# Attention tiles turned in 32x32 blocks on VectorE, one of six on TensorE, and the product with v in K=32 pieces

## The reference

```python
    q_bucket = np.sum(q_bits * powers, axis=-1)
    k_bucket = np.sum(k_bits * powers, axis=-1)
    mask = q_bucket[:, :, :, None] == k_bucket[:, :, None, :]
    scores = scale * np.matmul(q, k.transpose(0, 1, 3, 2))
    scores = np.where(mask, scores, -1000000000.0)
    scores = scores - np.max(scores, axis=-1, keepdims=True)
    attn = np.exp(scores)
    attn = attn / (np.sum(attn, axis=-1, keepdims=True) + 1e-09)
    return np.matmul(attn, v).astype(np.float32)
```

## Time and profile before

| | us |
|---|---|
| median of 3 runs (758.93 to 759.16) | 759.15 |
| the profiled execution | 759.28 |
| its span | 757.5 |
| TensorE busy | 747.0 (99%) |
| VectorE busy | 438.1 (58%) |
| ScalarE busy | 348.2 (46%) |
| GpSimd busy | 368.9 (49%) |

### The profile page before, as it was taken

One profiled execution on the slowest core, in us unless ns is written; L12 is line 12 of the kernel. 1 busy time (PEld: TensorE's weight loads), 2 busy tenths in 40 slices (PEclk: granted clock), 3 DMA queues, 4 the chain that ended last, 5 costly groups with the idle time before them and its releaser, 6 DMA issues.

```text
span 757.5 us, 12511 instructions
## 1 busy us (share of the span) xinstructions
PE 747.0 (99%) x4179; PEld 623.4 (82%) x4179; DVE 438.1 (58%) x858; ACT 348.2 (46%) x658; POOL 368.9 (49%) x253
## 2 busy tenths in 40 slices
PE   9999999999999999999999999999999999999996
PEld 7677777777776888888888888998899889889985
DVE  8777777777765745565555656597157027414710
ACT  7766677777764233432433310375057017404700
POOL 5966567878820799998978830253200120010001
PEclk9999999999999999999999999999999999999999
DMA  4434323212111799887886702510200010000000
GB/s 110 135 95 116 98 77 96 69 50 68 27 47 27 267 312 319 283 263 240 275 286 197 273 23 84 195 43 0 71 15 1 28 57 1 1 28 15 1 15 28
DMA packets 54301, 82.08 MB, mean 108 GB/s; under 512 B 21632, under 2 KB 33568, under 8 KB 54240
## 3 DMA queue, kind: packets, MB, share of 16 engines
q1 hardware_dynamic: 41152, 38.44, 16.8%
q10 hardware_dynamic: 9584, 31.53, 12.7%
q0 software_dynamic: 3504, 11.30, 4.6%
HBM read 64.67 MB, written 15.48 MB: 106 GB/s over the span
## 4 chain that ended last, share of the span: by engine, by line
PE 62%; issue 29%; POOL 3%; DVE 2%; ACT 2%; DMA 1%; SPq 0%; POOLq 0%; DVEq 0%
PE pair_s L1528 14%; PE pair_t L1543 14%; PE pair_u L1334 9%; PE bank_b L1349 8%; PE pair_s L1321 5%; PE pair_t L1321 4%; PE pair_u L1503 2%; PE bank_b L1374 2%; POOL out L682 1%; PE pair_s L1581 1%; DVE g_lo L1263 1%; PE pair_s L1454 1%; PE bank_a L1290 1%; POOL y_raw L676 1%; POOL w_part L550 1%
## 5 line engine op out<-in xcount | busy, mean ns | idle before, releaser
L550 POOL TENSOR_TENSOR w_part<-w_raw,w_part 128x1024 fp32r<-128x1024 f32 x80 | 190.5, 2404 | 45.9 <-ACT w_part L792 45.4
L792 ACT ACTIVATE w_part<-w_raw 128x1024 fp32r<-128x1024 f32 x72 | 76.3, 1060 | 117.8 <-DMA w_raw<-in_moe_w 102.9
L1630 PE MATMUL pair_t<-w_part,g_hi 128*128 128x512 f32 x384 | 119.0, 391 | 0.3 <-POOL w_part L550 0.3
L682 POOL DMA_INDIRECT out<-o_sb,token x12 | 11.8, 984 | 208.5 <-DVE o_sb L1233 208.5
L1528 PE MATMUL pair_s<-w_part,xs_t 128*128 x456 | 108.8, 394 | 0.2 <-issue 0.2
L1543 PE MATMUL pair_t<-w_part,hid_t 128*128 x456 | 107.1, 390 | 0.0
L1543 PEld LDWEIGHTS pair_t<-w_part,hid_t 128*128 128x128 f32 x456 | 85.4, 188 | 17.6
L1528 PEld LDWEIGHTS pair_s<-w_part,xs_t 128*128 128x128 f32 x456 | 84.3, 188 | 17.9 <-issue 0.9
L895 ACT ACTIVATE elu<-elu 128x384 f32<-128x384 f32 x64 | 33.6, 524 | 121.2 <-DVE elu L1253 121.1
L734 ACT ACTIVATE exps<-exps,nmax 128x768 f32<-128x768 f32 x96 | 88.5, 925 | 0.5 <-DVE exps L952 0.4
L1630 PEld LDWEIGHTS pair_t<-w_part,g_hi 128*128 128x128 f32 x384 | 71.6, 188 | 15.1 <-issue 0.7
(11 more groups left out here) (221 smaller groups left out, 1088.2 us busy)
## 6 DMA issues: line engine op xcount, KB each, us to landing
w_raw<-in_moe_w ACTq DMA_DIRECT2D x48, 512.0 KB, 3.9
w_raw<-in_moe_w SPq DMA_DIRECT2D x16, 512.0 KB, 8.1
ys_sorted<-ys SPq DMA_DIRECT2D x19, 256.5 KB, 6.4
x_sorted<-xs_raw SPq DMA_DIRECT2D x16, 256.0 KB
xs_q<-x_sorted SPq DMA_DIRECT2D x64, 64.0 KB, 4.7
w_raw<-in_moe_w_in ACTq DMA_DIRECT2D x8, 512.0 KB, 4.0
raw<-in_q SPq DMA_DIRECT2D x16, 192.0 KB, 3.2
raw<-in_k SPq DMA_DIRECT2D x16, 192.0 KB, 3.4
```

Of the source, the lines that this page charges most:

```text
L550: pool.tensor_tensor(chunk_of(w_part, n, 1, c), w_raw[n % 2][c][:, :], chunk_of(w_part, n, 0, c).bitcast(F32), ALU.subtract).then_inc(s_wl ...
L792: act.activation(chunk_of(w_part, n, 0, c), w_raw[n % 2][c][:, :], ACT.Copy).then_inc(s_whi, 1)
L1630: mm = pe.matmul(pair_t[:, t % 2, :], gp[:, f, j * P:(j + 1) * P], w_out_p[:, wp, f, :], start=f == 0 and m == 0, stop=f == FT - 1 and m == 2)
```

## The change

VectorE turns the first five tiles of each head itself, with one transpose instruction per tile, `turn(m)`, from `exps` to a new array `turned`. It transposes each 32x32 block in place, so that a partition holds key k of its block of 32 and every group of 32 partitions holds another quarter of the queries. The product with v therefore sums over 32 keys at a time: `times_v(u, first, end)` has for each pair of key blocks 4 row groups (one for each quarter, writing to a PSUM bank of its own) times 2 column groups, 96 products of K = 32 with 160 columns per head, in two pieces of 48 behind the first and the second score tile of the head two later. v is loaded four times per head in that layout (`v_quads`) and once as before.

The sixth tile is still turned by TensorE (`turn_alone`, into whichever score pair is free), copied whole by ScalarE (`copy_alone`), and multiplied by six products of 128 columns. In head 15 VectorE turns all six tiles, and the product comes in two parts (four tiles, two tiles). `last` has six products of 80 columns where it had three of 160. ScalarE takes over the rounding `high` for heads 3 and up, and no longer copies halves of turned tiles. Score pairs no longer alternate strictly, as `turn_alone` takes one in its turn. TensorE's scores are given tile by tile. The first product with v starts at m = 12, two heads behind the scores.

```diff
--- before.py
+++ after.py
+KEY_BLOCKS = S // 32
+PAIRS = KEY_BLOCKS // 2
+AV_AT = 512 - J * 32
+BLOCKED = J - 1
+ALONE_AT = AV_AT + 32 - P
...
-            v_nat = sb("v_nat", [P, 4, J, D])
             exps = sb("exps", [P, 4, S])
-            exps_t = sb("exps_t", [P, J, 4 * HALF])
+            turned = sb("turned", [P, 2 * BLOCKED + 1, S])
...
+            v_quads = sb("v_quads", [P, 3, KEY_BLOCKS * D])
+            v_nat = sb("v_nat", [P, 3, J, D])
...
+        quad = ctx.enter_context(nc.psum_tensor("quad", [P, 4, 512], F32))
         pair_s = ctx.enter_context(nc.psum_tensor("pair_s", [P, 2, 512], F32))
         pair_t = ctx.enter_context(nc.psum_tensor("pair_t", [P, 2, 512], F32))
-        pair_u = ctx.enter_context(nc.psum_tensor("pair_u", [P, 2, 512], F32))
+        bank_a, bank_b, pair_u = quad[:, 0, :], quad[:, 1, :], quad[:, 2:4, :]
...
+        scored = lambda m: score_pair[use_of(m) % 2]
+        alone = lambda h: score_pair[(use_of(J * (h + 1) + JH - 1) + 1) % 2]
+        first_turned = lambda u: 512 - blocked(u) * 32
+        out_pair = lambda u: pair_t if u == HEADS - 2 else quad[:, 1:3, :]
...
             def load_v(g):
-                if g >= 4:
+                if g >= 3:
                     sp.wait_ge(s_av, g - 2)
-                sp.dma_start(v_nat[:, g % 4], rows(v, g)).then_inc(s_vld[g % 4], 16)
+                for i in range(4):
+                    sp.dma_start(v_quads[i * 32:(i + 1) * 32, g % 3, :].rearrange("k (p n) -> k p n", p=4),
+                                 quad_rows(v, g)).then_inc(s_vld[g % 3], 16)
+                if g < HEADS - 1:
+                    sp.dma_start(v_nat[:, g % 3], rows(v, g)).then_inc(s_vld[g % 3], 16)
...
+            def high(g, c):
+                at = (slice(0, D), slice(D, P))[c]
+                if c == 0:
+                    act.wait_ge(s_raw[g % 2][0], 16 * (g // 2 + 1))
+                else:
+                    act.wait_ge(s_ks, g)
+                act.wait_ge(s_sc, J * (g - 2))
+                act.activation((q_b, k_b)[c][at, g % 3, :], raw[at, g % 2, :], ACT.Copy).then_inc(s_hr, 1)
...
             def copy_u(u):
                 act.wait_ge(s_av, u + 1)
-                if u >= 2:
-                    act.wait_ge(s_fin, u - 1)
-                act.activation(u_sb[:, u % 2 * HALF:(u % 2 + 1) * HALF], u_bank(u)[:, 0:HALF], ACT.Copy).then_inc(s_u, 1)
+                if u >= 1:
+                    act.wait_ge(s_fin, u)
+                if u == HEADS - 1:
+                    act.activation(kept_u[:, 0:2], turned_u(quad[:, 0:2, :], u), ACT.Copy).then_inc(s_u, 1)
+                else:
+                    act.activation(kept_u[:, :, 0:BLOCKED], turned_u(quad, u), ACT.Copy)
+                    act.activation(u_sb[:, BLOCKED * P:], quad[:, 3, ALONE_AT:ALONE_AT + P], ACT.Copy).then_inc(s_u, 1)
+
+            def copy_alone(h):
+                act.wait_ge(s_pt, h + 1)
+                if h >= 1:
+                    act.wait_ge(s_av, h)
+                act.activation(turned[:, 2 * BLOCKED, :].rearrange("p (o n) -> p o n", o=2), alone(h)[:, :, 0:HALF],
+                               ACT.Copy).then_inc(s_tt, 1)
...
+            for m in range(J, J * HEADS):
+                g, i = m // J, m % J
+                exp_rows(m)
+                if i == 0:
+                    if g == 2:
+                        big_bits(3)
+                    if g + 2 < HEADS and g >= 2:
+                        high(g + 2, 0)
+                if i == 1:
+                    if g == 1:
+                        big_bits(2)
+                        high(3, 0)
+                    if g >= 2:
+                        copy_u(g - 2)
+                    copy_alone(g - 1)
+                if i == 2 and g >= 2:
+                    copy_rows(g - 2)
+                if i == 3 and g + 2 < HEADS:
+                    high(g + 2, 1)
+                if i == 4 and 2 <= g < HEADS - 2:
+                    big_bits(g + 2)
+                if i >= 4 and 7 <= g < 7 + NCH:
+                    first_hi(g - 7, i - 4)
...
-            def copy_t1(m):
-                hh = m // JH
-                if hh >= 4:
-                    dve.wait_ge(s_av, (hh - 1) // 2)
-                dve.wait_ge(s_pt, 2 * m + 2)
-                dve.tensor_copy(turned_tile(m, slice(JH, J)),
-                                exps_pair(m)[:, 1, 0:HALF].rearrange("p (j n) -> p j n", j=JH)).then_inc(s_t1, 1)
+            def turn(m):
+                g, qt = place_of(m)
+                dve.wait_ge(s_ex, m + 1)
+                if g >= 2 and qt == 0:
+                    dve.wait_ge(s_av, g - 1)
+                if qt == BLOCKED:
+                    dve.wait_ge(s_av, g)
+                dve.transpose(turned[:, place_turned(g) + qt, :], exps[:, m % 4, :]).then_inc(s_tn, 1)
...
+            for m in range(J, J * HEADS):
+                g, i = m // J, m % J
+                least(m)
+                if m == 2 * J - 1:
+                    sign(3)
+                if i == 3 and 2 <= g < HEADS - 2:
+                    sign(g + 2)
+                if (m - 2) % J < BLOCKED:
+                    turn(m - 2)
+                if m == J + 1:
+                    sign(2)
+                if i == 1:
+                    inverse(g - 1)
+                if m == 2 * J + 2:
                     dve.wait_ge(s_cst, 16)
                     dve.tensor_copy(tri_bf[:, :], cc("tri"))
                     dve.tensor_copy(ones_bf[:, :], cc("ones"))
+            turn(J * HEADS - 2)
+            turn(J * HEADS - 1)
+            inverse(HEADS - 1)
...
+                if g >= 1 and qt == JH + 1:
+                    pe.wait_ge(s_tt, g)
+                elif m >= 2:
+                    pe.wait_ge(s_mx, m if g >= 1 and qt == JH else m - 1)
...
-            def turn_exps(m):
-                if m == 0:
-                    pe.wait_ge(s_sgn, 2)
-                pe.wait_ge(s_ex, m + 1)
-                for part, free in enumerate((s_t0, s_t1)):
-                    if 1 <= m < J * HEADS - 2:
-                        pe.wait_ge(free, m)
-                    for n in range(JH):
-                        kt = part * JH + n
-                        mm = pe.transpose(exps_pair(m)[:, part, n * P:(n + 1) * P], exps[:, m % 4, kt * P:(kt + 1) * P],
-                                          ident)
-                    mm.then_inc(s_pt, 1)
-
-            def times_v(u, half):
-
-                if half == 0:
-                    pe.wait_ge(s_t0, min(J * u + JH, J * HEADS))
-                    pe.wait_ge(s_t1, min(J * u + JH, J * HEADS))
-                    if u < HEADS:
-                        pe.wait_ge(s_vld[u % 4], 16 * (u // 4 + 1))
+            def turn_alone(h):
+                pe.wait_ge(s_ex, J * (h + 1))
+                pe.wait_ge(s_mx, J * (h + 1) + JH - 1)
+                for n in range(J):
+                    mm = pe.transpose(alone(h)[:, n // JH, n % JH * P:(n % JH + 1) * P],
+                                      exps[:, (J * h + BLOCKED) % 4, n * P:(n + 1) * P], ident)
+                mm.then_inc(s_pt, 1)
+
+            def times_v(u, first, end, tiles=slice(0, BLOCKED)):
+
+                if first == 0:
+                    pe.wait_ge(s_tn, BLOCKED * u + tiles.stop)
+                    pe.wait_ge(s_vld[u % 3], 80 * (u // 3 + 1) - (16 if u == HEADS - 1 else 0))
+                    pe.wait_ge(s_sgn, min(u + 4, HEADS))
+                    if u >= 1:
+                        pe.wait_ge(s_u, u)
                     if 1 <= u < HEADS - 1:
                         pe.wait_ge(s_fr, u)
-                for j in range(half * JH, (half + 1) * JH):
-                    for o in range(2):
-                        mm = pe.matmul(u_bank(u)[o * D:(o + 1) * D, 0:HALF], v_nat[:, (u - 1 + o) % 4, j, :],
-                                       turned_half(2 * u - 1 + o)[:, j], start=j == 0, stop=j == J - 1)
-                if half == 1:
+                if first == 0 and u < HEADS - 1:
+                    pe.wait_ge(s_tt, u + 1)
+                    for j in range(J):
+                        o = j % 2
+                        pe.matmul(quad[o * D:(o + 1) * D, 3, ALONE_AT:ALONE_AT + P], v_nat[:, u % 3, j, :],
+                                  turned[:, 2 * BLOCKED, j * P:(j + 1) * P], start=j < 2, stop=j >= J - 2)
+                to = slice(first_turned(u) + tiles.start * 32, first_turned(u) + tiles.stop * 32)
+                at = slice(place_turned(u) + tiles.start, place_turned(u) + tiles.stop)
+                for i in range(first, end):
+                    for r in range(4):
+                        rows = slice(r * 32, (r + 1) * 32)
+                        for o in range(2):
+                            key = 2 * i + o
+                            a = (key % 4 * J + key // 4) * D
+                            mm = pe.matmul(quad[o * D:(o + 1) * D, r, to], v_quads[rows, u % 3, a:a + D],
+                                           turned[rows, at, key * 32:(key + 1) * 32],
```

(34 more changed lines are left out.)

330 lines of the change are left out of this document (95 added, 235 removed).

## The result

| | us |
|---|---|
| kernel before, median of 4 runs (758.93 to 759.33) | 759.15 |
| changed kernel, median of 4 runs (776.43 to 780.96) | 777.8 |
| ratio, 95% interval | 1.025 (1.0237 to 1.0262) |
| profiled execution of the changed kernel, its span | 777.1, 775.3 |

The change makes the kernel 2.5% slower. The forecast was 761.4 with a range of 742 to 782: sign and range hold the result. The mechanism doesn't. VectorE was to become the bound, and it didn't.

What follows compares the result with a forecast made beforehand. TensorE's stream bounded the kernel before, and VectorE was to bound it after. Start +3.7, +2.7 by the last tile, tail -0.5: net +2.2 on 759.28 gives 761.5, median 761.4 us; range 742 to 782.

Steps and rivals of the forecast that it cites:

- VectorE's transpose: Each block transpose of 128x768 on VectorE steps 1.56 us, bounds 1.52 to 1.67; five per head make 7.80 of 13.83.
- The start: Heads 0 and 1, before head 2's first read: nine transposes on VectorE that can't be hidden, +3.7 us.
- TensorE's work: TensorE per head: 11.3 us with changes of shape, if the eight places of the K = 32 products run side by side.
- The fast-transpose rival: VectorE's contiguous transpose costs a plain read's 0.885 us; period 11.8, time 722; chance 0.10.
- The wait of sign on project: Fourth tile of a head: VectorE's sign waits 0.25 us for project, 2.69 against VectorE's own 2.45.
- SyncE "issues four more loads per head, far ahead of their use": SyncE's queue: four added loads per head come far ahead of their use; no wait was priced for them.
- The clock: TensorE's clock might fall in the first 12 tiles; the first pieces would cost about 2 us, inside the bounds.
- Supply of instructions: TensorE's issue limit in the product with v: 0.028 us a pass, 192 passes making 5.4 us per head.
- The tail: From the last tile to r_m: 10.45 us where before needs 10.95, so -0.5 us.
- the period forecast (14.08): Each head takes 14.08 us, 0.1 less than before, with VectorE setting the pace.
- its own sign of being wrong: A mean of the new VectorE transpose under 1.5 us makes the forecast wrong on the faster side.
- The second rival: TensorE's row groups don't run side by side: 6.6 us per head gives 796, 5.4 gives 782; chance 0.16.

Runs made afterwards that it cites:

- e8: Changed kernel with 24 extra VectorE block transposes in six forms at the end of attention; 512 columns took 701 ns contiguous, 1108 with stride 4, 727 writing PSUM.
- e10: e1 with SyncE issuing the eight mask loads before, not behind, the loads of q and k, from head 5's loads on; 764.2 us.
- e13: e11 with e6's edit, so VectorE turns all six tiles of a head; 750.0 us.
- e11: e10 with the four short pieces of the product with v from e5; 762.8 us.
- e4: Changed kernel with project ahead of last, instead of behind it, in the fourth tile of a head; 783.5 us.
- e6: e1 with VectorE turning all six tiles of a head, the tile turned on TensorE, its copy and its own product gone; 769.3 us.
- e1: Changed kernel with the five loads of v(0) moved in front of head 2's mask loads on SyncE's queue; 772.5 us.
- e14: e13 with v(1) loaded before head 4's q and k, gate weights behind them, and expert-weight pieces two heads later; 745.1 us.
- e5: e1 with the K = 32 products from head 3 on in four pieces of 24 products instead of two of 48; 772.0 us.
- e9: Changed kernel with v(0) as early as in e1, gate weights and first expert-weight piece behind head 4's q and k, later pieces one head later; 776.8 us.
- e2: Changed kernel where all K = 32 products but the first key pair's compute 32 of 160 query columns, their number unchanged; 788.9 us.

## Why the prediction was right or wrong, step by step

- **VectorE's transpose**, the term on which the sum rested: 1.56 us a step expected, 0.90 measured. The row it came from the earlier trace rows reads with stride 4, and that layout makes 1.11 of 0.70 us (e8). The prediction named the stride as what could put it lower and gave it to a rival of 0.10; the row was the nearest by name of the instruction, and not by its layout. VectorE's 13.83 per head was 3.3 too much.
- **The start**, +3.7 at head 2's first read: -1.2 measured. It had nine transposes at 1.56. With 0.90 each it is 5.9 less, -2.2; the remaining 1.0 is in waits and small terms that it had put too low.
- **TensorE's work**, 11.3 per head: 12.2 (e10). Six score tiles take 5.0 and not 4.5 (0.78 to 0.90 each, the upper values behind a change of shape), the pieces 3.68 and not 3.3, `last` 1.39 and not 1.26, the sixth tile's own product 0.81 and not 0.65. That the eight places run side by side was right, with a piece at 1.84 where I had 1.65. The Trainium skill (TensorE: Matmul & The Clock Gate, Part 3) states strict order of starts and ends; by it the prediction had priced 6.6 per head, and the 3.68 measured disagree with that reading.
- **The fast-transpose rival** put the period at 11.8 once the transpose was a plain read's. Its condition came true and its period didn't: 13.5 in the best heads of e10, and 14.2 in heads 4 to 11 of the changed kernel. It added one exposed wait to VectorE's sum. In the trace TensorE's 12.2 stand in a chain with two reads of VectorE between (0.50 and 0.77), since the tile turned on TensorE holds a score pair and `sign`, a transpose and a read stand between `project` and the next pair. With no tile turned on TensorE, and the pieces spread, the period was 11.9 (e13); with the pieces spread alone it was 13.3 (e11).
- **The wait of sign on project**, 0.25 expected: 11.1 us in 11 heads, 1.0 each. Most of this follows from the transpose: with 0.90 in the prediction's own sum the wait is 2.69 less 1.79, 0.9, and with the mask loads out of the way it is still 0.8 a head (e10, 9.1 in 11). Close behind stood a chain of which the prediction said nothing, GpSimd's k, SyncE's loads of q and k, eight mask loads; it takes over when `project` comes sooner (e4) or the head gets shorter (e6).
- **SyncE "issues four more loads per head, far ahead of their use"**: this is the sentence that failed most. v(0) was 4.44 us late, head 4's q 7.46, and head 2 lost 10.5 us by them and by the clock. I had counted the loads and not walked the queue of the first heads, in which a load stands behind waits. Of the 10.5, e1 gave back 4.6; e14's 15.7 is 1.4 above a head of before, and still 3.8 above its own heads of 11.9.
- **The clock**: "about 2, inside these bounds". The mean of 0.63 from 20 to 40 us was in fact behind several of the terms of head 2, and I can't part it from the loads: e14 still has 0.66 there and head 2 in 15.7, but its clock is back at the upper level at 36.2 us and the changed kernel's only at 42.3.
- **Supply of instructions** was in the prediction only as 0.028 us a pass. Passes of 32 columns take 11.5 ns, and the cost is that of a late packet: breaks of 0.3 to 1.7 us in four heads from 60 to 220 us, 3.2 in all, and 1.65 in the tail. The prediction had no term for a late packet.
- **The tail**, -0.5 expected, +3.1: 192 passes of 128 columns took 4.6 us with their break of 1.28 (I had 2.6) and 192 of 64 columns 2.9 with one of 0.37 (1.4). Without the breaks that is 17 and 13 ns a pass, where I had let the time fall with the columns to 14 and 7. Head 15 lost 3.3, where a full product with v stands before the last reads; the forecast's 11.07 there lacked it, and with half of that product moved ahead head 15 takes 11.4 (e5, e11).

That sign and range hold the result is luck. An error of some 3.3 us per head too much on VectorE stood against several too little elsewhere, so that the period forecast (14.08) lies beside the one measured in heads 4 to 11 (14.22) for another reason; and of the 18.0 us lost, 16.9 lie in head 2, head 15 and the tail, where the forecast's whole net was +2.2. By its own sign of being wrong, a transpose under 1.5, it should have been wrong on the faster side. That no step but the places side by side came out at its number is the fair summary. (The second rival's terms add up to 795, not 796.)

What stays open: why e9's later heads were slower than e1's, why packets are late in the single long heads of e13 and e14, and how much of head 2 is the clock alone. Runs of one of these kernels also lie 2 to 10 us apart, where the kernel before has 0.4 to 1.6; packets that are late in some executions and not in others would do that, but no run parts it.

## What to carry to other kernels

A duration carries over only with its access pattern: compare stride, target and shape before the name of the instruction. When work goes over into many small products, ask three things that busy time doesn't show: what a pass of few columns still costs, when the next packet of instructions arrives and what large transfers run at that moment, and what the clock does with the columns taken away. And a load that is "far ahead" is so only if the queue in front of it is, in the first heads too: here the order of SyncE's queue alone was worth 13.6 us (777.8 to 764.2).

## What the runs showed of the hardware

- A block transpose of f32 at 1.04 ns per column and lane when contiguous, 1.6 times as long when it reads every fourth column; writing PSUM from contiguous columns costs 4% (e8).
- Products with K = 32 in eight places side by side: 96 passes of 160 columns in 1.84 us, of 192 in 2.14 (e6), of 32 in 1.10 (e2). With the tail's two widths, breaks taken off, a pass takes 11.5, 13.4, 17.2, 19.2 and 22.3 ns at 32, 64, 128, 160 and 192 columns; an estimate through the first and the fourth is 9.6 ns and 0.06 per column.
- TensorE's instructions move in packets of 16 KB that share the DMA engines with data. Where those were 98.9% busy the packet came 1.9 us into a piece, and the next piece broke off; a broken piece went on 1.2 to 1.7 us behind the end of the packet (in e1 at 113.22, the packet from 110.6 to 111.5; in e2 at 106.13, the packet from 103.7 to 104.7).
- Taking columns from TensorE put its granted clock from 0.98 to 0.85 on average from 60 to 220 us, and the kernel came out 11 us slower (e2).
